# Numerator products of linear attention: the tail tokens of two heads share one tile (Trainium2, one core)

## What is computed

```python
def phi(x):
    proj = einsum('bhsd,df->bhsf', x, w_phi)
    proj = proj - max(abs(proj), axis=-1, keepdims=True)
    return concatenate([exp(proj), exp(-proj)], axis=-1)      # 256 features
q_p, k_p = phi(q), phi(k)
kv = einsum('bhsf,bhsd->bhfd', k_p, v);  z = sum(k_p, axis=2)
num = einsum('bhsf,bhfd->bhsd', q_p, kv)
den = einsum('bhsf,bhf->bhs', q_p, z)[..., None] + 1e-06
attn = num / den
```

## Time and profile before

| | |
|---|---|
| median of 3 executions | 1040.98 us |
| lowest, highest | 1039.56, 1041.26 us |
| the profiled execution's own time | 1041.62 us |
| its span, first to last instruction | 1039.3 us |
| PE, PEld busy | 1026.1 (99%), 948.6 (91%) us |
| DVE, ACT, POOL busy | 661.2 (64%), 592.7 (57%), 368.7 (35%) us |
| PE instructions of line 390 (numerator) | 640, 74.4 us |
| PE instructions of line 376 (kv) | 576, 69.5 us |

### The profile page before, as it was taken

How to read it: one execution, slowest core, us unless ns; L and a number is a source line. 1 busy time by engine, 2 the same in 40 slices (tenths; PEclk the granted TensorE clock), 3 DMA queues, 4 the chain that set the end, 5 groups by cost and what they waited for, 6 DMA issues and landing times.

```text
span 1039.3 us, 17321 instructions
## 1 busy us (share of the span) xinstructions
PE 1026.1 (99%) x6129; PEld 948.6 (91%) x6129; DVE 661.2 (64%) x1156; ACT 592.7 (57%) x1036; POOL 368.7 (35%) x365
## 2 busy tenths in 40 slices
PE   8999999999998999999999999999999999999998
PEld 7999999999988899899899899899899899899897
DVE  5675776798974657665585565855567555674443
ACT  5776566676645556555555666565655665644341
POOL 5622433254152426232351333523343323631210
PEclk9999999999998999999999999999999999999999
DMA  5233121220143231233223232233225223232101
GB/s 153 60 90 90 36 69 46 59 47 13 57 117 102 62 92 62 82 92 102 67 66 102 62 92 72 71 92 102 62 71 159 65 91 102 61 122 82 61 2 61
DMA packets 101314, 80.32 MB, mean 77 GB/s; under 512 B 56944, under 2 KB 81776, under 8 KB 101232
## 3 DMA queue, kind: packets, MB, share of 16 engines
q1 hardware_dynamic: 100992, 78.91, 26.8%
q10 hardware_dynamic: 240, 0.33, 0.1%
HBM read 66.10 MB, written 4.72 MB: 68 GB/s over the span
## 4 chain that ended last, share of the span: by engine, by line
PE 94%; DMA 2%; DVE 1%; POOL 1%; ACT 1%; SPq 1%; issue 0%; DVEq 0%; ACTq 0%; POOLq 0%
PE bank L1135 37%; PE bank L1112 33%; PE bank L390 6%; PE bank L376 6%; PE bank L338 4%; PE bank L359 3%; PE bank L622 2%; PE bank L642 2%; PE bank L332 1%; DMA rawqk<-qkT 1%; DMA st_w<-w1a 1%; DMA xT_high_halves<-xn 0%; DVE amax_q L440 0%; ACT feat_k L470 0%; DVE shift_q L451 0%
## 5 line engine op out<-in xcount | busy, mean ns | idle before, releaser
L1135 PE MATMUL bank<-w2op,hid 128*128 128x512 f32 x1728 | 426.9, 392 | 1.2 <-DVE w2op L1356 1.2
L1135 PEld LDWEIGHTS bank<-w2op,hid 128*128 128x128 f32 x1728 | 321.8, 188 | 58.5 <-issue 1.8
L1112 PE MATMUL bank<-x_T,w1op 128*128 128x384 f32 x1152 | 211.3, 339 | 3.6 <-ACT part_a L1370 3.6
L1112 PEld LDWEIGHTS bank<-x_T,w1op 128*128 128x128 f32 x1152 | 204.2, 190 | 7.7 <-issue 4.0
L1112 PE MATMUL bank<-x_B,w1op 128*128 128x384 f32 x864 | 173.5, 336 | 0.0
L1112 PEld LDWEIGHTS bank<-x_B,w1op 128*128 128x128 f32 x864 | 154.2, 188 | 11.3
L1307 POOL TENSOR_TENSOR w_sums<-st_w 128x256 f32<-128x256 f32 x48 | 49.4, 1028 | 227.9 <-DVE w1op L1343 222.5
L1415 DVE SCALAR_TENSOR_TENSOR hid<-part_s,hid 128x384 fp32r<-128x384 f32 x141 | 98.0, 722 | 37.3 <-ACT hid L1411 37.1
L1356 DVE TENSOR_TENSOR w2op<-st_w,w2op 128x1024 fp32r<-128x1024 f32 x48 | 64.9, 1355 | 46.6 <-ACT w2op L1352 46.6
L1275 POOL TENSOR_TENSOR x_sums<-xraw 128x256 f32<-128x256 f32 x30 | 22.3, 767 | 203.1 <-ACT xraw L1227 125.2
L1411 ACT ACTIVATE hid<-part_s 128x384 fp32r<-128x384 f32 x141 | 73.4, 525 | 32.0 <-DVE part_s L1385 31.6
(11 more groups left out here) (179 smaller groups left out, 1609.1 us busy)
## 6 DMA issues: line engine op xcount, KB each, us to landing
st_w<-w1a SPq DMA_DIRECT2D x24, 512.0 KB, 3.4
st_w<-w2a SPq DMA_DIRECT2D x24, 512.0 KB, 3.8
st_w<-w1b SPq DMA_DIRECT2D x24, 512.0 KB, 3.4
st_w<-w2b SPq DMA_DIRECT2D x24, 512.0 KB, 3.7
v<-v SPq DMA_DIRECT2D x16, 256.0 KB, 3.1
out<-xall SPq DMA_DIRECT2D x16, 256.0 KB, 2.1
rawqk<-qkT SPq DMA_DIRECT2D x14, 288.0 KB, 4.0
rawqk<-qkT SPq DMA_DIRECT2D x14, 256.0 KB, 3.7
```

The costliest lines, as they stand in the source:

```text
L1112: last = nc.tensor.matmul(dst, w1op[g % 2][:, a, W1OP.index(w), c, :], xop[x][:, b, c, :], start=name in ("M2", "M1", "M7") and k_ == 0, s ...
L1135: last = nc.tensor.matmul(acc[t0 + t][:, :], hid[name, g % 2][:, x, P * t:P * (t + 1)], w2op[g % 2][:, y, j, :], start=first and k_ == 0, ...
```

## The change

The numerator of each head has 8 products in place of 10. The first head's turn has two more, one for each feature half, on a tile of its own, `qfT_tails`, that holds the transposed tail block of both heads; the moving operand is kv of both heads, `kv[:, :, f, :]`, 2 pieces of 65 columns. The result goes to columns 260 to 390 of the first head's bank: rows 0 to 63 of the first 65 columns are head 0's tail, rows 64 to 127 of the second 65 head 1's. The other two quarters are not read. The finish of the first head has 6 columns of den and four tail pieces, the finish of the second 4 columns and none. The copy of round 4 has the same 256 columns and goes to `qfT_tails`.

```diff
-    qfT, o = at("qfT", [P, 2, 2, S], F32, o)
+    qfT, o = at("qfT", [P, 2, 2, MT * P], F32, o)
+    qfT_tails, o = at("qfT_tails", [P, 2, 2 * TAIL], F32, o)
...
         for f in range(2):
             if a == 0:
                 pe.wait_ge(kv_copied, 2 * g + f + 1)
-            for n in list(range(MT + 1))[::-1 if f else 1]:
-                r0 = P * n if n < MT else S - P
+            for n in list(range(MT))[::-1 if f else 1]:
                 last = nc.tensor.matmul(psN[a][:, (D + 1) * n:(D + 1) * (n + 1)],
-                                        qfT[:, a, f, r0:r0 + P], kv[:, a, f, :],
-                                        start=f == n == 0, stop=f == 1 and n == 0)
+                                        qfT[:, a, f, P * n:P * (n + 1)], kv[:, a, f, :],
+                                        start=f == n == 0, stop=a == 1 and f == 1 and n == 0)
+        if a == 0:
+            for f in range(2):
+                last = nc.tensor.matmul(psN[0][:, (D + 1) * MT:(D + 1) * (MT + 2)].rearrange("p (h c) -> p h c", h=2),
+                                        qfT_tails[:, f, :], kv[:, :, f, :], start=False, stop=f == 1)
         last.then_inc(num_done, 1)
...
-            src = psT[:, 0:2 * P].rearrange("p (f a c) -> p a f c", a=2, f=2)
-            dst = qfT[:, :, :, MT * P:S]
+            src = psT[:, 0:2 * P].rearrange("p (f c) -> p f c", f=2)
+            dst = qfT_tails[:, :, :]
...
+        tiles = MT if a else MT + 2
...
-        for s_ in range(2):
-            rows = slice(TAIL + T2 * s_, TAIL + T2 * (s_ + 1))
-            last = nc.vector.tensor_scalar(xall[0:T2, 4 + s_, b, cols], nd[rows, MT, 0:D], rden[rows, MT:MT + 1],
-                                           None, ALU.mult)
+        if a == 0:
+            for h, s_ in ((0, 0), (0, 1), (1, 0), (1, 1)):
+                rows = slice(TAIL * h + T2 * s_, TAIL * h + T2 * (s_ + 1))
+                last = nc.vector.tensor_scalar(xall[0:T2, 4 + s_, b, c + D * h:c + D * (h + 1)], nd[rows, MT + h, 0:D],
+                                               rden[rows, MT + h:MT + h + 1], None, ALU.mult)
         last.then_inc(fin, 1)
```

More of the change, by code:

```diff
@@ L141, in program @@
     kv, o = at("kv", [P, 2, 2, D + 1], F32, o)
-    den, o = at("den", [P, MT + 1], F32, o)
-    rden, o = at("rden", [P, MT + 1], F32, o)
-    qfT, o = at("qfT", [P, 2, 2, S], F32, o)
+    den, o = at("den", [P, MT + 2], F32, o)
+    rden, o = at("rden", [P, MT + 2], F32, o)
+    qfT, o = at("qfT", [P, 2, 2, MT * P], F32, o)
+    qfT_tails, o = at("qfT_tails", [P, 2, 2 * TAIL], F32, o)
     for part in ("hi", "lo"):
@@ L498, in dve_finish @@
         need(dve, fin, n)
-        nd = psN[a][:, 0:(MT + 1) * (D + 1)].rearrange("p (t c) -> p t c", t=MT + 1)
-        nc.vector.tensor_scalar(den[:, :], nd[:, :, D], EPS, None, ALU.add).then_inc(den_done, 1)
+        tiles = MT if a else MT + 2
+        nd = psN[a][:, 0:tiles * (D + 1)].rearrange("p (t c) -> p t c", t=tiles)
+        nc.vector.tensor_scalar(den[:, 0:tiles], nd[:, :, D], EPS, None, ALU.add).then_inc(den_done, 1)
         dve.wait_ge(den_done, n + 1)
-        nc.vector.reciprocal(rden[:, :], den[:, :]).then_inc(rden_done, 1)
+        nc.vector.reciprocal(rden[:, 0:tiles], den[:, 0:tiles]).then_inc(rden_done, 1)
         dve.wait_ge(rden_done, n + 1)
@@ L505, in dve_finish @@
         cols = slice(c, c + D)
-        nc.vector.tensor_tensor(
+        last = nc.vector.tensor_tensor(
             xall[:, 0:4, b, cols].rearrange("p (t s) c -> p s t c", s=2),
```

## The result

| | before | changed |
|---|---|---|
| median of 5 executions | 1040.53 us | 1035.25 us |
| lowest, highest | 1039.56, 1041.26 | 1034.85, 1035.86 |
| profiled execution, span | 1041.62, 1039.3 | 1035.32, 1033.5 |

The ratio is 0.9949 with a 95% interval of 0.9938 to 0.9961: 5.3 us faster, 4.1 to 6.5.

What follows compares the result with a forecast made beforehand. TensorE with its weight loads was taken to bound attention: 7.1 us saved over 16 pairs, less losses of 0.44, 0.44, 0.23 and 0.1, gives 5.9 us. Forecast median 1035.1 us, range 1032.3 to 1037.2.

Steps and rivals of the forecast that it cites:

- The bound and the price: Attention numerators: TensorE and its weight loads are full, 0.111 us per instruction at either width, so a pair saves 0.44 us.
- rival B: Numerator products: time grows with the columns, so no saving exists; 1041 us, chance 0.03.
- C: Wide tail products: the two-piece operand is worked as two, 0.36 us each; 8.8 us slower, 1049.8 us, chance 0.02.
- DVE's sum is unchanged: Both heads' finishes: four tail pieces of 0.29 us move to the first turn; the pair's sum stays the same.
- The finish costs nothing: First head's finish: 0.58 us longer, but covered by the 2.9 us before the next kv; cost nothing.
- Loss 1, the input loop: Third transposes wait for input loads: 0.23 us lost in slot 3, 0.1 in slots 2, 4, 5, 6, 10 together.
- rival A: Input loop: inputs land half a us later, so five plain slots lose 2.1 us more; 1037.2 us, chance 0.09.
- Loss 2, slot 14: Slot 14: PE already idles there for the input DMA, so slot 13's numerator saving is lost, 0.44 us.
- Loss 3, slot 13: Last transposes of slot 13: the stall grows by up to 0.44 us but ends in slot 14's slack; no second loss.
- Loss 4, the last pair: After the last pair: PE's second sine product waits for DVE's split, so that pair's 0.44 us is lost.
- The MLP moves forward whole: Behind attention: the chain up to 315 us and the 720 us of MLP move forward whole, the wait keeping its length.
- Rival D, the half clock: 24 products after the wait ending at 315.14 us: without the lower clock, 2.8 us less, 1032.3 us, chance 0.08.

Runs made afterwards that it cites:

- mirrored change: The changed kernel with the two wide products behind the second head's eight, in that head's bank, and the pieces in its finish: 1036.10 us; with early inputs 1035.54 us.

## Why the prediction was right, point by point

**The bound and the price.** Right. A pair saves 0.45 us (0.44 forecast), as a wide instruction costs 0.112 us. The run with two narrow products gives all of the gain back, the run of 65 columns gives nothing more, so rival B (time grows with the columns) and C (the operand in two pieces costs) are out. The bound of 0.07 us for each was not needed, though one of the four does pay it: the second wide one starts 0.169 us behind the first, and the four take 0.50 us, 0.125 each, which is over the 0.12 that the prediction named as a sign of being wrong. The narrow group behind them gives it back, and in the mirrored change, where none follows, it stays as 0.05 us a pair. In slots 7 and 11, where Fourier products of the second step stand around and between the numerators, the stretch is only 0.38 us shorter (slot 11: 9.44 us before, from 180.05 to 189.49, and 9.06 now, from 176.36 to 185.42); the prediction took 0.44 for every pair, and no run shows what keeps the rest. The isolated gap of the Trainium skill, "TensorE: Matmul & The Clock Gate", section "Back-to-back issue gap", which grows with the moving columns, did not hold for these products with a weight load each: the spacing is 0.112 us at 65 and at 130 columns.

**DVE's sum is unchanged.** Off by 0.26 us a pair, in the kernel's favour (0.19 by the busy sum, 3.0 us over 16 pairs). From the first finish's first operation to what follows both finishes DVE takes 2.75 us in slot 7 (102.58 to 105.33) and took 3.01 in the trace before (104.75 to 107.76). What stands behind a finish's large multiplication now starts 0.08 us before its recorded end: the four pieces in the first finish (103.33, the multiplication ending at 103.41), the next operation in the second. The pieces before started 0.02 us behind it. So the first finish grew by 0.47 us and not 0.58, and the second shrank by 0.73.

**The finish costs nothing.** Wrong as put, right in the sum. The 2.9 us of cover is that of a plain slot. In slots 7 and 11 DVE comes late and kv waits 0.2 us for it; PE had to wait for DVE at a later projection unit in these slots anyway, and the shift is 2.22 us behind slot 7's wait and was 2.17 ahead of it.

**Loss 1, the input loop.** The mechanism was right, the size too small and the slots partly others: 0.23 in slot 3 and 0.1 elsewhere were forecast, 0.40 and 0.30 (slot 10) were lost in the first trace, and about 1.7 us of waits stand in the second. The two runs with early inputs remove it. The room was read from one trace; that PE's wait at one slot scatters by 0.9 us, one trace could not tell. This is rival A in part, but not by later landings, as it had them: SP's issue of a v load ahead of the q and k loads took 1.02 and 1.96 us in slot 10, with flights of 3.62 and 3.63.

**Loss 2, slot 14.** Wrong. 0.44 us were to be lost, since PE idled there already. The changed kernel does not wait there and gains 0.3 us instead. The wait belonged to that execution: ahead of those q and k loads one issue of a v load took 1.25 us in the trace before, and the flight was an ordinary one:

```profile
215.43 1.25 SPq L545
...
218.11 3.76 DMA rawqk<-qkT
```

The run with two narrow products, whose numerators are as long as before, does not wait there either.

**Loss 3, slot 13.** The stall grew, by 0.05 us where up to 0.44 was allowed for. It was to end in the slack of slot 14, and there is none in this trace: the shift goes from 4.51 us at slot 13 to 4.91 at slot 14, 0.40 and not 0.45. So it is a loss, a small one.

**Slot 15**, 0.18 us, was not in the list. Its third transposes wait for a chain of DVE's finishes and three copies on ACT that start from Fourier work, as the chain of waits of the changed kernel has it:

```profile
238.37 0.72 ACT xall L665 x2
...
239.49 0.50 ACT qfT L489
...
240.03 0.66 PE bank L360 x4
```

**Loss 4, the last pair.** Mis-sized: 0.16 us lost and not 0.44, PE's wait there being 0.28 us and not 0.57, because on just this path DVE's two finishes got 0.19 us shorter (3.06 us before, from 267.80 to 270.86, and 2.87 now, from 261.76 to 264.63) and began 0.11 us closer behind kv.

**The sum.** Forecast were 5.9 us and a time of 1035.1; measured were 1035.25 and, the second time, 1036.35, both in the range of 1032.3 to 1037.2. At the last kv group the shift is 5.93 us, at the last Fourier product 6.23, at the end 5.79. The steps' errors cancel in part: the input loop and slot 15 cost 0.55 us more than counted, slot 14 and the last pair 1.0 less. Attention gained 0.3 us more than forecast, and the wait at 315 us took it back. The price per pair was understood; that the time came within 0.2 us of the forecast is luck in part, the more so as the second measurement lies 1.2 us above it.

**The MLP moves forward whole.** Nearly. The wait that ends at 315 us was to keep its length. Measured from start to start it was 3.96 us before and 4.52 in the change, and it goes from 3.96 to 4.87 in the thirteen traces, of which the trace before has the shortest. Nothing ties it to the change: the kernels that only differ in attention are spread over the whole range.

**Rival D, the half clock.** In no trace did the slow stretch vanish, but its length differs. The 24 products behind the wait take 6.86 us in the change and 5.97 in the first run with early inputs:

```profile
308.49 5.97 PE L1118 MATMUL bank<-x_T,w1op 128*128 128x384 f32 x24 [3.80 <-ACT part_a L1376]
```

The thirteen traces have 5.96 to 7.09 us. So the price of this rival is 1.1 us at most, not 2.8.

## What to carry to other kernels

Where each matmul brings its own weight load, count instructions and not columns, as far as the trace bears it out (here up to 130 columns; products of 384 columns stand 0.174 us apart): two products on the same stationary tile are best made as one with a wider moving operand, even if that is in two pieces. Then look for the transfer that the shortened work used to cover, and for what its issue stands behind, and take the room ahead of each wait from more than one execution. And before work is moved from one head's turn to the other's, ask which semaphore frees the buffer that it reads.

## What the runs showed of the hardware that was not expected

- SP's issue of one load, 0.60 or 0.67 us in most slots, took 1.02 us in one execution and 1.96 in another at the same slot of the same kernel (slot 10), while the flight of the loads behind it stayed at 3.6 us. PE waited 0.25 and 1.14 us for it.
- Around a wait of 3.96 to 4.87 us the granted clock was at the lower of its two levels, 1.2 GHz, for a part of the next products in all thirteen traces; the same 24 products took from 5.96 to 7.09 us, so this place alone moves an execution by 1.1 us.
- A group of narrow fp32 products is 0.06 us shorter behind wide ones than behind narrow ones: 16 take 1.73 us behind the wide tail products, 1.79 behind the narrow ones. The wide group ahead is 0.05 us longer for it (0.50 against 0.45).
